# A fused attention and two-MLP kernel: another order of work inside an attention step, and the attention tensors laid out anew

## The reference

```python
# q, k, v: (4, 8, 576, 64); s: (4, 8, 576)
scores = q @ k^T / sqrt(64)
cum    = cumsum(maximum(s, 0), axis=-1)
scores = where(causal, -1e9, scores + minimum(-(cum_i - cum_j), 0))
attn   = exp(scores - rowmax); attn /= sum(attn) + 1e-9
x      = (attn @ v) as (2304 tokens, 512)
h = x @ w_in                    # 512 -> 2048
x = (h - tanh(h)) @ w_out       # 2048 -> 512
h = x @ w2_in                   # 512 -> 1024
solu = h * softmax(h)
out = layernorm(solu) * g_ln @ w2_out    # 1024 -> 512
```

## Time and profile before

| | us |
|---|---|
| median of 3 runs | 853.44 (853.18 to 853.65) |
| the profiled execution | 852.49 |
| its span | 850.7 |
| busy PE / PEld | 819.1 / 706.8 |
| busy DVE / ACT / POOL | 452.0 / 398.9 / 126.9 |
| mean granted TensorE clock | 0.994 |

### The profile page before, as it was taken

The page is one execution under the profiler, slowest core; times in us unless marked ns, Lnnn a source line. Parts: engine busy times, 40 slices in busy tenths (PEclk is TensorE's granted clock), DMA queues, the critical chain, the costliest instruction groups (busy, mean ns, idle before and its releaser), DMA issues.

```text
span 850.7 us, 14122 instructions
## 1 busy us (share of the span) xinstructions
PE 819.1 (96%) x4552; PEld 706.8 (83%) x4552; DVE 452.0 (53%) x1059; ACT 398.9 (47%) x888; POOL 126.9 (15%) x150
## 2 busy tenths in 40 slices
PE   6899999998899999999999999999999999999998
PEld 5778777777788888888888888899988888888886
DVE  4888889889764342224222422333647544555452
ACT  3989989989653332223222322233623433333323
POOL 2244243343100000000000000000022212221210
PEclk8999999999999999999999999999999999999999
DMA  6554555553353300000000000000300000000001
GB/s 160 140 155 112 141 144 126 147 126 96 115 161 102 118 4 1 1 1 0 0 0 0 0 0 0 0 1 1 99 0 1 26 25 25 25 25 12 25 25 38
DMA packets 77714, 46.29 MB, mean 54 GB/s; under 512 B 59824, under 2 KB 68144, under 8 KB 77680
## 3 DMA queue, kind: packets, MB, share of 16 engines
q1 hardware_dynamic: 76432, 45.49, 19.1%
q10 hardware_dynamic: 1248, 0.37, 0.2%
HBM read 40.97 MB, written 4.87 MB: 54 GB/s over the span
## 4 chain that ended last, share of the span: by engine, by line
PE 82%; DVE 6%; issue 5%; ACT 4%; DVEq 0%; POOL 0%; ACTq 0%; POOLq 0%
PE psum L1141 23%; PE psum L1154 23%; PE psum L1352 12%; PE psum L1380 11%; PE psum L1238 3%; PE psum L1196 3%; DVE probs L951 2%; PE psum L1267 2%; PE psum L1366 2%; ACT probs L701 2%; DVE pT_lo L934 1%; ACT x_low L728 1%; PE psum L1200 1%; DVE qkT_lo L982 1%; ACT qkT_hi L711 1%
## 5 line engine op out<-in xcount | busy, mean ns | idle before, releaser
L1141 PE MATMUL psum<-x_hi,w1i 128*128 128x464 f32 (+1 forms) x640 | 185.5, 371 | 1.7 <-DVE w1i L880 1.7
L1154 PE MATMUL psum<-gate_hi,w1o 128*128 128x464 f32 (+1 forms) x640 | 146.2, 370 | 0.0
L1141 PEld LDWEIGHTS psum<-x_hi,w1i 128*128 128x128 f32 x640 | 119.8, 188 | 16.2 <-DVE w1i L880 2.1
L1154 PEld LDWEIGHTS psum<-gate_hi,w1o 128*128 128x128 f32 x640 | 120.1, 188 | 13.5
L914 DVE TENSOR_TENSOR gate_lo<-gate,gate_hi 128x464 fp32r<-128x464 f32 (+1 forms) x80 | 51.2, 640 | 134.9 <-ACT gate_hi L671 134.9
L1141 PE MATMUL psum<-x_lo,w1i 128*128 128x464 f32 (+1 forms) x320 | 118.9, 372 | 0.0
L671 ACT ACTIVATE gate_hi<-gate 128x464 fp32r<-128x464 f32 (+1 forms) x80 | 47.1, 588 | 142.5 <-PE psum L1154 136.8
L904 DVE TENSOR_TENSOR gate<-psum,gate 128x464 f32<-128x464 f32 (+1 forms) x80 | 50.9, 636 | 99.6 <-ACT gate L660 99.6
L660 ACT ACTIVATE gate<-psum 128x464 f32<-128x464 f32 (+1 forms) x80 | 44.3, 553 | 109.7 <-PE psum L1141 104.5
L1380 PE MATMUL psum<-w2o,lnT_hi 128*128 128x512 f32 x288 | 92.2, 401 | 0.5 <-DVE lnT_lo L1097 0.5
L701 ACT ACTIVATE probs<-probs,neg_max 128x128 f32<-128x128 f32 (+2 forms) x144 | 83.9, 583 | 11.4 <-DVE neg_max L951 9.1
(11 more groups left out here) (109 smaller groups left out, 1225.6 us busy)
## 6 DMA issues: line engine op xcount, KB each, us to landing
cum_bc<-cum_dram SPq DMA_DIRECT2D x16, 576.0 KB, 4.7
rden_T<-rden_dram SPq DMA_DIRECT2D x32, 144.0 KB, 3.1
out_x<-out_sb SPq DMA_DIRECT2D x18, 256.0 KB, 2.0
stage<-in_q SPq DMA_DIRECT2D x32, 128.0 KB, 2.3
v_raw<-in_v SPq DMA_DIRECT2D x32, 128.0 KB, 3.7
stage<-in_moe_w_in SPq DMA_DIRECT2D x16, 256.0 KB, 3.1
stage<-in_moe_w_out SPq DMA_DIRECT2D x16, 256.0 KB, 3.5
stage<-in_k SPq DMA_DIRECT2D x30, 128.0 KB, 2.4
```

The costliest lines, as they stand in the source:

```text
L1141: mm = pe.matmul(h_ps[j % 4][:, 0:wide(c)], wp[j][:, kt, :], xp[:, kt, 0:wide(c)], start=(n == 0), stop=(n == 3 * KT - 1))
L1154: mm = pe.matmul(y_ps[m][:, 0:wide(c)], wp[j][:, m * P:(m + 1) * P], gp[j % 2][:, 0:wide(c)], start=(j == 0 and wp is w1o_hi and gp is gat ...
```

## The change

- **A slot on PE:** `turn_qk(0)` moves ahead of `score(2)`, and `turn_rden` behind `turn_p("A3")`. `attend(-1, 0, 0)` waits also for `rden_rows`, since 1/sum is now turned into the bank in which x begins (bank 6); the wait of `turn_rden` for `qk_lo` goes.
- **A slot on ACT:** `rden_rows_copy` moves behind `p_hi("A3")`, and its wait for `turn_qk(0)` goes; `qk_copy(2)` moves ahead of `p_hi("B2")` and `exp(1, 3)`.
- **A slot on DVE:** `x_add(0)` moves behind two biases, `denominators` behind two more; `qk_rest(2)` and the tail's bias move ahead of `p_lo("B2")`, the bias now behind `qk_rest(2)`.
- **Slot 0:** the tail's score and `score(2)` come ahead of all three turns, and ACT and DVE follow that order.
- **DMA:** k of pair 1 is issued on ACT's queue (three DMAs) and not on SP's.
- **x split:** parts 0 to 2 are split in slot 15, each where q, k of the next pair would be; part 3 in slot 16 behind A2.
- **Layout:** the tensors needed last (sums, v, `pT_lo`, `rden_T`, `x_low`, `x_sum`) lie where w_in tiles come; the others lie under w_out. The pad goes. ACT waits for `attended` at j = 4 and for `x_done` at j = 9 of the first chunk.

```diff
+            pT_hi = sb("pT_hi", [P, 2, PT_W], F32R)
+            v_parts = [sb(f"v_parts{n}", [P, NT, 4 * D], F32R) for n in range(2)]
...
+            w1i_words = GATE_W + FT * 2 * DM
+            sb("gap", [P, w1i_words - sum(attention_words)])
+            cum_bc = [sb(f"cum_bc{n}", [P, 2, S]) for n in range(2)]
...
-        rden_ps = qk_ps[0:TILES, TAIL + P:TAIL + 2 * P]
+        rden_ps = bank(6)[0:TILES, 0:P]
...
-        FIRST_ORDER = ORDER[:4] + ORDER[8:] + ORDER[4:8]
+        FIRST_ORDER = ORDER[:6] + ORDER[8:] + ORDER[6:8]
...
                 if sl.fixed and sl.s == -1:
-                    load_qk(1, 1)
+                    load_tokens(sp, q_raw[1], q_pairs, 1, qk_in[1], diagonal=True)
...
             act.activation(row_sum[0][:, 0:1], ident[:, 0:1], ACT.Exp)
+            act.wait_ge(dve_const, 2)
+            load_tokens(act, k_raw[1], k_pairs, 1, qk_in[1])
...
-            def first_x(sl):
-                if sl.fixed and sl.s in (PAIRS - 2, PAIRS - 1):
+            def first_x(sl, kt):
+                if sl.fixed and sl.s == (PAIRS if kt == KT - 1 else PAIRS - 1):
                     act.wait_ge(x_done, HALVES)
-                    split_x(0, (0, 1) if sl.s == PAIRS - 2 else (2, 3))
+                    split_x(0, (kt,))
...
                 if sl.fixed and sl.s == 0:
-                    exp(0, 0)
+                    for h in range(2):
+                        exp(h, 0)
+                        exp(h, 1)
                     qk_copy(0)
-                    exp(0, 1)
+                    exp(0, 2)
                     qk_copy(1)
-                    exp(1, 0)
-                    exp(1, 1)
+                    exp(1, 2)
                     qk_copy(2)
-                    for t in (2, 3):
-                        exp(0, t)
-                        exp(1, t)
+                    exp(0, 3)
+                    exp(1, 3)
                     exp(None, FULL)
...
                 exp(1, 1)
-                rden_rows_copy()
+                first_x(sl, 3)
                 qk_copy(0)
+                first_x(sl, 0)
                 first_w1i(sl, 0)
                 p_hi("A3")
+                rden_rows_copy()
                 exp(0, 2)
...
                 exp(0, 3)
                 first_w1i(sl, 2)
+                qk_copy(2)
+                first_x(sl, 2)
                 p_hi("B2")
                 exp(1, 3)
-                qk_copy(2)
                 first_w1i(sl, 3)
...
-            act.wait_ge(x_done, PAIRS)
             for j in range(1, FT):
+                if j == 4:
+                    act.wait_ge(attended, 2 * PAIRS)
+                if j == 9:
+                    act.wait_ge(x_done, PAIRS)
                 step(0, j)
...
-                x_add(0)
                 bias(0, 0)
                 bias(0, 1)
-                denominators()
+                x_add(0)
                 p_lo("A01")
                 bias(1, 0)
                 bias(1, 1)
+                denominators()
                 p_lo("A2")
...
                 bias(1, 3)
+                qk_rest(2)
+                first_x(sl, 2)
+                bias(None, FULL)
                 p_lo("B2")
-                bias(None, FULL)
-                qk_rest(2)
...
                                 wait(pe, x_added, 2 * pair)
+                                pe.wait_ge(rden_rows, pair + 1)
...
                     score(0, 1)
+                    score_tail()
+                    score(2)
                     turn_qk(0)
-                    score_tail()
                     turn_qk(1)
-                    score(2)
                     turn_qk(2)
                     score(3)
...
                 turn_p("A2")
+                turn_qk(0)
                 score(2)
-                turn_rden()
-                turn_qk(0)
                 attend(-2, 1, 0)
                 turn_p("A3")
+                turn_rden()
                 attend(-2, 1, 1, 2, 3, 4)
```

More of the change, by code:

```diff
@@ L124, in build_transformer @@
             sb = tensors(phase, attention_words)
-            probs = [sb(f"probs{n}", [P, PW]) for n in range(2)]
             qkT_hi = [sb(f"qkT_hi{n}", [P, QK_W], F32R) for n in range(2)]
             qkT_lo = [sb(f"qkT_lo{n}", [P, QK_W], F32R) for n in range(2)]
-            cum_bc = [sb(f"cum_bc{n}", [P, 2, S]) for n in range(2)]
-            cum_tail = sb("cum_tail", [P, S])
-            v_raw = [sb(f"v_raw{n}", [P, NT, 2 * D]) for n in range(2)]
+            probs = [sb(f"probs{n}", [P, PW]) for n in range(2)]
+            pT_hi = sb("pT_hi", [P, 2, PT_W], F32R)
+            v_parts = [sb(f"v_parts{n}", [P, NT, 4 * D], F32R) for n in range(2)]
             ident_b = sb("ident_b", [P, P], BF16)
@@ L138, in build_transformer @@
             den = [sb(f"den{n}", [P, TILES]) for n in range(2)]
-            early_words = sum(attention_words)
             rden = [sb(f"rden{n}", [P, TILES]) for n in range(2)]
+            rden_row = sb("rden_row", [TILES, P])
+            w1i_words = GATE_W + FT * 2 * DM
+            sb("gap", [P, w1i_words - sum(attention_words)])
+            cum_bc = [sb(f"cum_bc{n}", [P, 2, S]) for n in range(2)]
+            cum_tail = sb("cum_tail", [P, S])
+            v_raw = [sb(f"v_raw{n}", [P, NT, 2 * D]) for n in range(2)]
+            pT_lo = sb("pT_lo", [P, 2, PT_W], F32R)
             rden_T = [sb(f"rden_T{n}", [P, S]) for n in range(2)]
-            rden_row = sb("rden_row", [TILES, P])
-            v_parts = [sb(f"v_parts{n}", [P, NT, 4 * D], F32R) for n in range(2)]
             x_low = sb("x_low", [P, S])
             x_sum = sb("x_sum", [P, S])
-            pT_hi = sb("pT_hi", [P, 2, PT_W], F32R)
-            pT_lo = sb("pT_lo", [P, 2, PT_W], F32R)
         warm_b = x_sum[:, 0:P // 2].bitcast(BF16)
@@ L161, in build_transformer @@
         behind_words = AHEAD * 2 * KT * P
-        before = FT * 2 * DM + 6 * CH
-        pad = -(-max(sum(attention_words) + 64 - (before + FT * 2 * KT * P - behind_words), 8) // 8) * 8
+        before = GATE_W + FT * 2 * DM
+        pad = 0
+        assert sum(attention_words) <= before + FT * 2 * KT * P - behind_words
         with ExitStack() as phase:
@@ L718, in rden_rows_copy @@
                         wait(act, rden_out, 32 * pair)
-                        if sl.runs(1):
-                            act.wait_ge(turned_qk, 3 * sl.pair(1)[0] + 1)
                         act.activation(rden_row[:, :], rden_ps, ACT.Copy).then_inc(rden_rows, 1)
@@ L764, in slot @@
                 qk_copy(1)
+                first_x(sl, 1)
                 exp(1, 2)
@@ L989, in slot @@
                         bias(1, t)
+                    bias(0, 2)
+                    bias(1, 2)
                     qk_rest(0)
@@ L1021, in slot @@
                 bias(1, 3)
+                qk_rest(2)
+                first_x(sl, 2)
+                bias(None, FULL)
                 p_lo("B2")
-                bias(None, FULL)
-                qk_rest(2)
                 first_w1i(sl, 3)
                 p_lo("B3")
-                first_x(sl)
             attention(dve, slot)
@@ L1293, in turn_rden @@
                         pe.wait_ge(den_step, 2 * (pair + 1))
-                        wait(pe, qk_lo, 3 * (pair + 2) if sl.runs(1) else 3 * PAIRS)
                         wait(pe, rden_rows, pair)
```

6 lines of the change are left out of this document (2 added, 4 removed).

## The result

The kernel after takes 841.86 us (median of 4 runs, 841.43 to 842.06), that of before beside it 853.31 (4 runs, 852.35 to 853.65): ratio 0.9867, 95% interval 0.985 to 0.9884. The forecast was 840.6 with a range of 837.5 to 847.0. The profiled execution took 841.88, its span is 840.1.

What follows compares the result with a forecast made beforehand. Attention steps were taken as bound by hand-overs between three nearly full engines, the MLPs by PE. Gains of 4.8 (steps), 3.1 (start), 2.8 (end of attention) and 2.1 (hand-over), 12.8 in all, took 853.44 to 840.6 us; range 837.5 to 847.

Steps and rivals of the forecast that it cites:

- The steady step: Slots 2 to 14: step of 12.99 us computed to fall to 12.58; 0.37 taken for each of 13, 4.8 us.
- the hoists: Head of a steady step: x_add(0) behind two biases and turn_qk(0) ahead of score(2) win nothing, costed at +0.07 us.
- 1/sum later: Steady step: the later copy of 1/sum delays SP's stores and loads by 0.9 us; costed at nothing.
- SP's slack for k: Steady step: k lands at t = 13.9, its first user turn_qk(0) comes at 14.3; slack falls from 3.4 to 0.4 us.
- rival 3: Every step: q, k land late at turn_qk(0), making the kernel slower, 865 us; chance 0.05.
- The start: Slots 0 and 1: scores ahead of turns and k on ACT's queue; 3.1 us won, bounds 1.5 and 3.6.
- a sign of being wrong: Listed signs: PE waits for a DMA at turn_qk(0), tail's bias or p_lo("B2") ends last, bias (0, 0) passes 12.5.
- The end of attention: Slot 15's score to the first up: x split one by one wins 2.8 us, bounds 1.3 and 3.0.
- Slot 15 runs as a steady step and 0.15 us longer: 'A01' of slot 16 at 13.76: End of attention: slot 16's first transposes at t = 13.76, giving 17.77 us to the first up instead of 20.58.
- The hand-over: Into the first MLP: ACT waits for x_done at j = 9, so up(4) waits no more; 2.1 us, bounds 1.7 and 2.2.
- Rival 1: Steady step does not shorten because one of three close ends replaces the wait for qkT_lo; 845.4 us, chance 0.20.
- Rival 2: Ends give half: the sums' store is held up and the half clock stays at both ends; 843.7 us, chance 0.14.

Runs made afterwards that it cites:

- w_in tile first: Kernel after, with w_in's tile 4 split ahead of w_out's tiles 2 and 3 on ACT and DVE in the last step before up(4); 840.96 us.
- x's part 1 apart: Kernel after, with DVE's low part of x's part 1 moved from slot 15 to the head of slot 16; 841.77 us.
- last turn late: Kernel after, with the last q, k copy and rest (qk_copy(2), qk_rest(2)) put back where they were before; 848.57 us.
- no hoists: Kernel after, with turn_qk(0) back behind score(2) and x_add(0) back ahead of the first two biases; 846.11 us.
- before with two moves: Kernel before, with only x_add(0) behind the first two biases and the last q, k turn's copy and rest early; 850.97 us.
- filled kernel: Kernel after, turn_qk(0) behind score(2), w_in's tile 4 split first, pair 2's q, k loaded before v, plus unread matmuls where PE idles; 839.69 us.

## Why the prediction was right, and where it was off

**The steady step.** The forecast step was 12.58 us, and 12.57 was measured (163.36 / 13). From the last turn on, PE's own work sets the end, as forecast: in the step shown, the turn comes at t = 8.83 (forecast 8.98), and the next score 3.62 us behind it (3.60). The tail's bias and `p_lo("B3")`, for which the prediction had margins of 0.23 and 0.15 us, were done 0.33 and 0.31 ahead. PE's wait ahead of `turn_qk(2)` did not grow to 0.5 but stayed at 0.29. The term was mis-sized because I took 0.37 for a computed 0.41: measured 0.44 x 13 = 5.77 for 4.8.

The reason given for the hoists was wrong, though. "Everything up to `qk_rest(1)` moves by +0.07 and nothing is won here" fixed every time to the score. Undoing both moves costs 0.45 a step. What comes over from the step before (`x_low`, and with it `x_add(0)`) does not move with the score: when the step shortens by 0.4 at its end, that work is 0.4 later in t, and the order at the head of the step must leave it room. "1/sum later", "costed at nothing", is needed as well: without it a step gives 0.08 of the 0.44. So the size of the step was right, and the share given to each move was not. That was luck in part: the forecast was for all the moves together, and none of its steps asked what the step would be with one of them left out.

**SP's slack for k** was given as 0.4 us. It is there, and too thin for the issues of k that take about 1 us longer in slots 4 and 5: PE waits in slot 5 or 6 of each profiled execution with this order, which costs 0 to 0.85 us in all. So rival 3 decides in one step and not in all, and "costed at nothing" was wrong by up to that for the turn's hoist, which gives nothing for it.

**The start** gave 2.36 for 3.1. Bias (0, 2) came at 14.37, not 13.43: `score(2)` ran at half clock (12 to 14 us, 0.50), the mask behind it too, and `cum_bc` came 0.22 later. The score of slot 1 is then at 18.83 for 18.26. Where the clock fell only later, that score came at 18.11 to 18.38 in nine traces and at 18.50 in a tenth, so the reordering itself was sized well. Slot 1 lost 0.43 where I had it win 0.2: the wait of 1.58 for k, a DMA wait at `turn_qk(0)`, which the prediction named as a sign of being wrong. "DMA engines at a share of 1.06, so a second queue brings no bandwidth" held, and the rest of that term did not: the second queue brought nothing that can be measured. Here the Trainium skill ("DMA: Bandwidth & Descriptors", "Issuing engines are not separate DMA queues") agrees with the run.

**The end of attention** gave 0.98 for 2.8, within none of its bounds. Two steps failed. "Three parts, each about as long" as those of q and k: the low part beside POOL took 1.55, and PE idled for 1.14 and 1.12 us in slot 15. "Slot 15 runs as a steady step and 0.15 us longer: 'A01' of slot 16 at 13.76" is where it shows: with a full clock, in "w_in tile first", "A01" comes at t = 14.62 (208.47 against the score at 193.85), behind DVE's last `pT_lo`. So even at full clock the stretch is 17.70 us, 2.0 less than before, with a half clock in that of before. And the half clock stayed, a little earlier than before: 1.0 more. That was the reason for the lower bound of 1.3, but the bound took only one of the two. The held instruction makes the second idle stretch and not the first ("x's part 1 apart"); a kernel whose low parts all lie clear of POOL wasn't tried, so how much of the 0.8 us it would bring stays open.

The prediction set the row of 2.08 us of waiting for DVE and the clock behind it against the Trainium skill's sentence on DVE's copies ("TensorE: Matmul & The Clock Gate", "Loop structure matters more than you think"). The later runs lean to the side of the trace and do not settle it: with matmuls in the waits for DVE the mean clock is 0.998 or more in five of five executions, but four traces with the same waits unfilled have 1.00 there too.

**The hand-over** gave 1.31 for 2.1. "The chain ends at 239.9 and PE waits no more" took the w_out splits at 1.28 us. They took 2.27, since the same edit had put them beside POOL. With the w_in tile first the full 2.1 is there.

**The rivals.** Rival 1 (the step does not shorten) did not come about, and three kernels show how near it was: "last turn late", "no hoists" and "before with two moves". Rival 2 (the ends give half) was right in its place: the ends and the start together gave 4.65 for 8.0. Its cause was in part another, POOL beside DVE. The steady step paid back 1.0 of it, and so the median is 1.3 above the forecast. Of profiled executions it is 2.2, 841.88 for 839.7. That the total came so near is partly luck: 3.4 us missing at the start and the end were half made up by a term that was too small and by the 0.95 us between the profiled execution of before and its median.

## What to carry to other kernels

When a loop of full engines is to be shortened, fix the times of the work carried over from the turn before, not those relative to its first instruction, and ask of each part of the new order what the step would be without it. Ask of each edit which instructions it puts beside each other on DVE and POOL, not only on one queue. And where two versions differ by about 1 us, compare executions, and stretches of their traces, with the same granted clock before believing either median.

## What the runs showed of the hardware that I had not expected

**DVE waits out POOL.** A DVE instruction with both operands in SBUF that starts beside a TENSOR_TENSOR of POOL takes longer and ends behind POOL's end: low part of x, 1.55 for 0.64 (0.50 behind it); another, 1.91 (0.49 behind); two w_out splits, 2.27 for 1.28 (1.15 behind). What is left behind POOL's end is a little less than the instruction's usual time, so it is held and not slowed. Every trace here has such cases, that of before too, where it could have been read before the forecast (its split of a w_in tile takes 0.68 us elsewhere):

```profile
224.63 1.42 POOL L553 TENSOR_TENSOR xT<-x_sum,rden_T 128x576 f32<-128x576 f32 x1 [9.44 <-DVE x_sum L964]
...
225.00 1.60 DVE L880 TENSOR_TENSOR w1i<-stage,w1i 128x512 fp32r<-128x512 f32 x1
```

DVE instructions that read PSUM were not held in these traces: in the step of the kernel after, `qkT_lo` at 104.87 takes its usual 0.69 inside POOL's split of v (104.53 to 106.10). Of those with one operand in SBUF, `den` was held in the filled kernel (1.35 for 0.16, 0.03 behind), while a TENSOR_SCALAR of 128x1 in the second MLP takes its 0.15 us with more than 0.7 us of POOL's TENSOR_TENSOR to come (627.82 in the kernel after). The Trainium skill says that of the port pair that VectorE and GpSimd share ("SBUF — State Buffer", "SBUF: two separate sides"): one side holds it for a whole instruction, the other blocks. The traces agree for the instructions named as held.

**The clock falls at another place in each execution.** The same kernel after had 0.50 at 12 and 206 us once, at 20 to 26 and 208 the next time. Each time a stretch with PE idle came first (for the stretch at 206 us, 1.14 and 1.12 us of idle), but the same idle time was also followed by 1.00. Executions of one kernel differ by 0.5 to 4.8 us here, and those at a lower mean clock are as a rule the longer ones (not so within the filled kernel); that the clock makes the whole difference was not shown.
